# Query maxima from the transposed features, injected by full-mode matmuls, with keys and features in one block

## The reference, cut to what matters

```python
def _attn_ref(q, k, v, w_phi):              # batch 8, heads 8, seq 576, head_dim 64, 128 features
    def phi(x):
        proj = np.einsum('bhsd,df->bhsf', x, w_phi)
        proj = proj - np.max(np.abs(proj), axis=-1, keepdims=True)
        return np.concatenate([np.exp(proj), np.exp(-proj)], axis=-1)
    q_p, k_p = phi(q), phi(k)
    kv = np.einsum('bhsf,bhsd->bhfd', k_p, v)
    z = np.sum(k_p, axis=2)
    num = np.einsum('bhsf,bhfd->bhsd', q_p, kv)
    den = np.einsum('bhsf,bhf->bhs', q_p, z)[..., None] + 1e-06
    return num / den
# then, per batch, on the [576, 512] result x (fp32):
#   xk = mu_k*x + (1-mu_k)*x_prev;  xr = mu_r*x + (1-mu_r)*x_prev
#   x = sigmoid(xr @ w_r) * (relu(xk @ w_k)**2 @ w_v)
# and a second block: h = relu(x @ w_in); three-tap convolution along seq; h*sigmoid(conv) @ w_out
```

## Time and profile before

| | |
|---|---|
| median of 3 runs | 1417.46 us (1412.54 to 1421.47) |
| profiled execution, its own time | 1417.62 us |
| its span | 1415.8 us, 26326 instructions |
| TensorE busy | 1360.0 us, 96% |
| VectorE busy | 672.6 us, 48% |
| ScalarE busy | 626.6 us, 44% |
| DMA | 78.60 MB, mean 56 GB/s |

### The profile page before, as it was taken

One profiled execution on the slowest core, in us unless ns is written; L12 is line 12 of the kernel. 1 busy time (PEld: TensorE's weight loads), 2 busy tenths in 40 slices (PEclk: granted clock), 3 DMA queues, 4 the chain that ended last, 5 costly groups with the idle time before them and its releaser, 6 DMA issues. The chain is left out here.

```text
span 1415.8 us, 26326 instructions
## 1 busy us (share of the span) xinstructions
PE 1360.0 (96%) x10368; PEld 1211.6 (86%) x10368; DVE 672.6 (48%) x1047; ACT 626.6 (44%) x1111; POOL 13.5 (1%) x18
## 2 busy tenths in 40 slices
PE   5879999999999999999999999998899999999998
PEld 4668899889888889888988888998788988998997
DVE  5444244334433624442544362451757556655753
ACT  3536345454352534545445353443444443433532
POOL 0000000000000000000000000000300000000000
PEclk9879999999999999999999999999999999999999
DMA  5411202202212120220221212030310210110101
GB/s 165 124 45 40 58 27 77 63 20 69 61 45 70 40 58 26 62 78 19 70 54 53 69 41 58 25 116 22 93 64 1 71 64 30 41 63 30 41 30 38
DMA packets 94579, 78.60 MB, mean 56 GB/s; under 512 B 64656, under 2 KB 72976, under 8 KB 93456
## 3 DMA queue, kind: packets, MB, share of 16 engines
q1 hardware_dynamic: 94480, 77.10, 18.2%
HBM read 57.75 MB, written 19.02 MB: 54 GB/s over the span
## 5 line engine op out<-in xcount | busy, mean ns | idle before, releaser
L472 PE MATMUL psm<-xk_hi,wk_hi 128*128 128x288 f32 x512 | 158.6, 310 | 15.1 <-issue 6.9
L969 PE MATMUL psh<-y_hi,win_hi 128*128 128x288 f32 x512 | 153.9, 301 | 13.4 <-ACT h L1054 9.0
L818 DVE TENSOR_TENSOR k_lo<-square,k_hi 128x288 fp32r<-128x288 f32 x128 | 58.7, 458 | 221.3 <-ACT square L683 221.3
L472 PE MATMUL psm<-k_hi,wv_hi 128*128 128x288 f32 x512 | 154.4, 302 | 0.0
L472 PE MATMUL psm<-xk_lo,wk_hi 128*128 128x288 f32 x512 | 153.7, 300 | 0.0
L472 PE MATMUL psm<-xk_hi,wk_lo 128*128 128x288 f32 x512 | 153.2, 299 | 0.0
L970 PE MATMUL psh<-y_lo,win_hi 128*128 128x288 f32 x512 | 152.2, 297 | 0.0
L971 PE MATMUL psh<-y_hi,win_lo 128*128 128x288 f32 x512 | 151.6, 296 | 0.0
L472 PE MATMUL psm<-k_lo,wv_hi 128*128 128x288 f32 x512 | 151.1, 295 | 0.0
L472 PE MATMUL psm<-k_hi,wv_lo 128*128 128x288 f32 x512 | 150.8, 295 | 0.0
L1112 DVE SCALAR_TENSOR_TENSOR conv<-h,taps,conv 128x576 f32<-128x576 f32 x64 | 55.2, 863 | 141.3 <-ACT conv L1056 141.3
(11 more groups left out here) (116 smaller groups left out, 2810.9 us busy)
## 6 DMA issues: line engine op xcount, KB each, us to landing
v_nat<-in_v SPq DMA_DIRECT2D x32, 320.0 KB, 3.6
qk<-in_q SPq DMA_DIRECT2D x32, 288.0 KB, 2.9
qk<-in_k SPq DMA_DIRECT2D x32, 288.0 KB, 3.2
den<-den_scr SPq DMA_DIRECT2D x64, 144.0 KB, 3.0
y_scr<-y SPq DMA_DIRECT2D x64, 144.0 KB, 1.8
y<-y_scr SPq DMA_DIRECT2D x8, 1152.0 KB, 5.5
out<-rows SPq DMA_DIRECT2D x32, 256.0 KB, 2.0
den_parts<-den_rows SPq DMA_DIRECT2D x128, 2.2 KB, 1.9
```

The source lines that it names most:

```text
L472: return nc.tensor.matmul(o, lhsT, rhs, start=first, stop=last)
L818: nc.vector.tensor_tensor(k2_lo[:, i, :], square[:, i % 2, :], k2_hi[:, i, :].bitcast(F32), ALU.subtract).then_inc(k2_lo_ready, 1)
L969: nc.tensor.matmul(o, wh, xh, start=first, stop=False, skip_group_check=True)
```

## The change

The queries are projected once. The step E (`features_and_keys`) makes the query projections with features on partitions for all 576 tokens (four fp32 matmuls) and the key projections (ten), alternating between the two 64-row halves. VectorE turns the query features in 32x32 blocks (`q_turn`, two transposes) and reduces them to partial maxima (`part_maxima`); one TensorE transpose (M) brings the partial maxima of each token together, and VectorE reduces again and splits in hi and lo (`split_maxima`). Four DMAs on SP (`load_maxima`) lay the result out as rows, and the step PICK subtracts them by four f32r matmuls that use all 128 rows. The copy of the maxima by ScalarE and the second projection are gone. DEN and NUM write into the banks of the query features, in chunks of 512 and 64 columns; the key projections and KV use the other two banks. The steps' planned costs and fills are new, and the first batch no longer runs ahead into the second.

The diff, cut to its core:

```diff
-ROWS = D + 2
+TOK = S // 32
...
-PE_NS = {"QP": 1100, "KP": 1100, "M": 550, "P0": 800, "P1": 800, "KV": 2240, "DEN": 1000, "NUM": 1950,
+PE_NS = {"E": 2800, "M": 150, "PICK": 700, "KV": 4500, "DEN": 1200, "NUM": 2200,
          "K": 1590, "K-": 1190, "K+": 400, "R": 1590, "V-": 1590, "V": 1590}
 
-FILL_NS = {"QP": 2200, "M": 1600, "P0": 3500, "P1": 2600}
-FIRST_FILL, LAST_FILL, RC_AFTER, DV_AFTER = 6000, 1600, 3500, 9000
+FILL_NS = {"E": 3600, "M": 3200, "PICK": 1600, "KV": 1500, "NUM": 2200}
+FIRST_FILL, RC_AFTER, DV_AFTER = 6000, 3800, 9500
...
-    steps = [("QP", 0)]
-    for p in range(PAIRS):
-        steps += [(s, p) for s in ("KP", "M", "EK", "P0", "KV", "P1", "DEN", "NUM")]
-        steps += [("QP", p + 1)] if p + 1 < PAIRS else []
-    return steps
+    return [(s, p) for p in range(PAIRS) for s in ("E", "M", "EK", "PICK", "KV", "DEN", "NUM")]
...
-        def ahead(s):
-            return [(s, 0, "next") if last else (s, p + 1)]
-
         def before(s):
             return [(s, p - 1)] if p else []
 
-        steps += [("M", p)] + before("RC") + [("P0", p), ("EK", p)] + ahead("QP")
-        steps += [("KV", p), ("P1", p)] + before("DV") + ahead("KP") + [("DEN", p), ("NUM", p)]
+        steps += [("M", p)] + before("RC") + [("EK", p), ("PICK", p), ("KV", p)] + before("DV")
+        steps += [] if last else [("E", p + 1)]
+        steps += [("DEN", p), ("NUM", p)]
...
-            if not (ran_ahead and step in (("QP", 0), ("KP", 0))):
-                emit(step)
+            emit(step)
             if with_moe:
                 fill(FILL_NS.get(s, 0))
-                if s == "DEN":
+                if s == "NUM":
...
+    Q0, K_TAIL, Q_MAX, Q1 = 0, BANK + D, BANK + D + 2 * F, 2 * BANK - D
+    CHUNKS = (((0, BANK), (BANK, S)), ((0, D), (D, S)))
...
-    def await_att_psum(eng, p, a):
+    def q_cols(h, p, a):
+        return att_psum(p, a)[:, (Q0, Q1)[h]:(Q0, Q1)[h] + S]
+
+    def k_tail(p, a):
+        return att_psum(p, a)[:, K_TAIL:K_TAIL + 2 * F].rearrange("p (h f) -> p h f", h=2)
+
+    def k_main():
+        return ps1[:].rearrange("p h (t f) -> p h t f", t=TT - 1)
+
+    def turned_max(p, a):
+        return att_psum(p, a)[:, Q_MAX:Q_MAX + P]
+
+    def await_q_psum(eng, p, a):
 
         if first_of(a):
-            await_(eng, den_copied, PAIRS, a, p - 1)
+            await_(eng, num_copied, PAIRS, a, p - 1)
         elif second_of(a) and p == 0:
-            eng.wait_ge(den_copied, PAIRS - 1)
+            eng.wait_ge(num_copied, PAIRS - 1)
         else:
-            await_(eng, den_copied, PAIRS, a, p)
-
-    def place(h, t):
-        return (H - 1) * h + t
-
-    def blocks(flat):
-
-        return bass.AP(flat.tensor, flat.offset, [flat.ap[0], (F * (H - 1), 2), (F, TT), (1, F)])
-
-    def halves(flat):
-
-        return flat.rearrange("p (b s) -> p b s", s=BANK)[:, 0:2, 0:HALF]
+            await_(eng, num_copied, PAIRS, a, p)
...
+        def load_maxima(p, a):
+
+            await_(sp, q_max_split_ready, PAIRS, a, p + 1)
+            await_(sp, features, PAIRS, a, p)
+            for h in range(2):
+                for part in range(2):
+                    row = 2 * h + part
+                    sp.dma_start(max_rows[row:row + 1, :].bitcast(F32), q_max_split[TOK * h:TOK * h + TOK, part, :].bitcast(F32)).then_inc(rows_loaded, 16)
+
...
+                if kind == "M":
+                    load_maxima(step[1], a)
...
-                if kind == "DEN":
-                    spread_den(step[1], of)
+                if kind == "NUM":
+                    spread_den(step[1], a)
                 if kind == "RC":
-                    repeat_den(step[1], of)
+                    repeat_den(step[1], a)
...
-        def project(i, p, a):
-
-            if i == 0:
-                await_att_psum(pe, p, a)
-            else:
-                await_(pe, q_max_ready, PAIRS, a, p + 1)
-            await_(pe, (q_loaded, k_loaded)[i][p % 2], 16 * (PAIRS // 2), a, 16 * (p // 2 + 1))
-            ps = att_psum(p, a)
-            for n in range(TT):
-                for h, t in ((0, (n - 1) % TT), (1, (n + 1) % TT)):
-                    own, b = slice(D * h, D * h + D), place(h, t)
-                    if (h, t) == (1, 0):
-                        await_(pe, shared_bank, 2 * PAIRS, a, 2 * p + i + 1)
-                    last = mm(ps[:, F * b:F * b + F], qk[own, p % 2, i, P * t:P * t + P], phi[own, :], True, True)
-                    if (h, t) == (0, TT - 1):
-                        last.then_inc(shared_bank, 1)
-            last.then_inc(k_projected if i else q_projected, 1)
+        def features_and_keys(p, a):
+
+            await_q_psum(pe, p, a)
+            await_(pe, kvz_copied, PAIRS, a, p)
+            await_(pe, q_loaded[p % 2], 16 * (PAIRS // 2), a, 16 * (p // 2 + 1))
+            await_(pe, k_loaded[p % 2], 16 * (PAIRS // 2), a, 16 * (p // 2 + 1))
+            tails, keys = k_tail(p, a), k_main()
+
+            def key_tile(h, t):
+                own = slice(D * h, D * h + D)
+                o = tails[:, h, :] if t == TT - 1 else keys[:, h, t, :]
+                return mm(o, qk[own, p % 2, 1, P * t:P * t + P], phi[own, :], True, True)
+
+            def feature_chunk(h, chunk, first):
+                own, cols = slice(D * h, D * h + D), slice(*CHUNKS[h][chunk])
+                return mm(q_cols(h, p, a)[:, cols], phi[own, :], qk[own, p % 2, 0, cols], first, False)
+
+            key_tile(0, TT - 1).then_inc(shared_bank, 1)
+            feature_chunk(1, 1, True)
+            feature_chunk(0, 0, True)
+            await_(pe, shared_bank, 3 * PAIRS, a, 3 * p + 1)
+            key_tile(1, TT - 1).then_inc(shared_bank, 1)
+            key_tile(0, 0)
+            key_tile(1, 0)
+            await_(pe, shared_bank, 3 * PAIRS, a, 3 * p + 2)
+            feature_chunk(0, 1, True).then_inc(shared_bank, 1)
+            key_tile(1, 1)
+            key_tile(0, 1)
+            await_(pe, shared_bank, 3 * PAIRS, a, 3 * p + 3)
+            feature_chunk(1, 0, False).then_inc(raw_features, 1)
+            for t in range(2, TT - 1):
+                for h in range(2):
+                    last = key_tile(h, t)
+            last.then_inc(k_projected, 1)
 
         def turn_maxima(p, a):
-            await_(pe, q_max_split_ready, PAIRS, a, p + 1)
-            await_(pe, num_copied, PAIRS, a, p)
-            for t in range(TT):
-                last = nc.tensor.transpose(ps1[0:ROWS, P * t:P * t + P],
-                                           q_max_split[:, t, :, :].rearrange("p h r -> p (h r)")[:, 0:ROWS].bitcast(F32), ident[:])
-            last.then_inc(max_turned, 1)
-
-        def feature_rows(n, p, a):
-
-            if n == 0:
-                await_(pe, max_rows_ready, PAIRS, a, p + 1)
-            else:
-                await_(pe, q_exp_ready, 2 * H, a, 4 * p + 2)
-            cols = slice(HALF * n, HALF * n + HALF)
+            await_(pe, q_part_ready, PAIRS, a, p + 1)
+            nc.tensor.matmul(turned_max(p, a), q_part[:], ident[:], start=False, stop=True, is_transpose=True,
+                             skip_group_check=True).then_inc(max_turned, 1)
+
+        def subtract_maxima(p, a):
+            await_(pe, rows_loaded, 64 * PAIRS, a, 64 * (p + 1))
+            await_(pe, k_tail_shifted, PAIRS, a, p + 1)
...
+                for chunk in CHUNKS[h]:
+                    cols = slice(*chunk)
+                    last = mm(q_cols(h, p, a)[:, cols], pick[:, h, :], max_rows[:, cols], False, True)
...
-                        last = mm(ps1[D * h:D * h + D, BANK * n:BANK * n + HALF], kvz[:, h, e, 0:D], q_exp[:, e, h, cols],
-                                  e == 0, e == 1)
+                        last = mm(q_cols(0, p, a)[D * h:D * h + D, cols], kvz[:, h, e, 0:D], q_exp[:, e, h, cols], e == 0, e == 1)
...
-        def exp_q(n, p, a):
-            await_(act, features, H, a, 2 * p + n + 1)
+        def exp_q(p, a):
+            await_(act, features, PAIRS, a, p + 1)
             await_(act, attended, PAIRS, a, p)
-            for e in range(2):
-                nc.scalar.activation(q_exp[:, e, :, HALF * n:HALF * n + HALF], halves(ps1[:]), ACT.Exp,
-                                     scale=1.0 - 2.0 * e).then_inc(q_exp_ready, 1)
+            for h in range(2):
+                for e in range(2):
+                    nc.scalar.activation(q_exp[:, e, h, :], q_cols(h, p, a), ACT.Exp, scale=1.0 - 2.0 * e).then_inc(q_exp_ready, 1)
...
-            await_(act, den_summed, PAIRS, a, p + 1)
+            await_(act, attended, PAIRS, a, p + 1)
             await_(act, den_spread, 64 * PAIRS, a, 64 * p)
-            nc.scalar.activation(two(den_rows[:]), halves(att_psum(p, a)[:, BANK:3 * BANK]), ACT.Copy).then_inc(den_copied, 1)
+            nc.scalar.activation(den_rows[:], q_cols(1, p, a), ACT.Copy).then_inc(den_copied, 1)
 
         def copy_num(p, a):
             await_(act, attended, PAIRS, a, p + 1)
             await_(act, x_ready, PAIRS, a, p)
```

(64 more changed lines are left out.)

122 lines of the change are left out of this document (51 added, 71 removed).

## The result

The changed kernel takes **1660.1 us** (median of 4, 1656.93 to 1669.47); the one before, beside it, 1419.1 (median of 4, 1412.54 to 1421.47). The ratio is 1.172 (that of the two medians 1.170), with a 95% interval of 1.166 to 1.178. The profiled execution took 1656.93, its span 1655.0: 239.2 over the 1415.8 of before. The forecast was 1556, its range ended at 1612. The direction came as forecast, and so did the waits for the row loads; the size did not, above all because the clock was also low behind the shorter waits, which the forecast left out.

A forecast was written before the change was run, and what follows sets the result against it. The prediction took TensorE's work, busy 96% of the span, as the bound. 1417.6 + 89 (stalls less saving) + 41 (clock) + 8 (first batch) = 1556 us, chance 0.42; range 1472 to 1612.

The forecast's parts named there:

- TensorE's saving: Matrix work per pair falls from 13.1 to 11.6 us: 1.5 saved (bounds 1.0 to 2.1), 6.0 per woven iteration.
- 2.8 that had run ahead: Second batch's QP0 and KP0 formerly ran ahead in the first batch, saving iteration 0 2.8 us that was counted twice.
- The stalls: TensorE waits in each woven iteration, mostly before PICK: 18.7 us; against 6.0 saved, 12.7 longer, +89 over seven.
- kvz: In pair 0, DEN directly follows KV and waits for the copy of kvz and hand-overs: 0.6 us.
- K+00: At a woven iteration's end TensorE reaches this tile before its inputs are ready: stall 2.1 us with the hand-over.
- The term c: Time of the four row loads from SP's start: 3.7 us, bounds 2.3 and 4.5; stalls sum to 4c + 3.9.
- M's own split is long done: In pair 1, the maxima are split well before SP can start the row loads, which end at 12.7 us.
- VectorE's work: New VectorE operations per pair: transposes 0.75 us each, partial maxima 1.35, main keys 1.22, key tail 0.42.
- The clock: Half clock follows only the stalls of pairs 1 and 3, 2.9 us each: 5.8 per woven iteration, +41.
- the first rival: Clock also falls after the shorter stalls: two more 2.9 us stretches per woven iteration, +41, 1597; chance 0.13.
- The first batch: It ends 5.6 us later, at 100.0; with the time counted twice, +8.4 in all (bounds -4 and +20).
- 22 per pair: First-batch pair: E's end to PICK 4.8 plus 3.7 us, PICK through E 11, waits behind weight pieces 2.5.

The follow-up runs named there:

- combined kernel: Changed kernel with two row loads, a retuned step list, 14 matmuls in each first-batch wait and a reordered first batch: 1404.2 us, ratio 0.992 to the kernel before.
- List B: Changed kernel with two row loads and a step list with four tiles between M and PICK in most pairs, none between PICK and KV: 1514.35 us.

## Why the prediction was right in kind and short in size

Against 1556, 1656.93 is 101 too much. The terms, each in turn:

- **TensorE's saving**: nearly right. Per pair in the woven part of after, group start to group start at full clock: E 2.77 (forecast 2.5), M 0.03 (0.1), PICK 0.79 (0.67), KV 4.38 (4.50), DEN and NUM 3.18 (3.3); 11.15 against 11.1. By busy time the woven part saved 31.5, where the forecast had 39.2 (42 less the 2.8 that had run ahead). In the second iteration of the combined kernel TensorE is busy for 111.25 against 116.51 of before, 5.3 less and not 6.0. The rest was not followed.
- **The stalls**: right in place, order and nearly in size. Forecast before the four PICKs 3.0, 5.9, 2.8, 4.3; measured in the second iteration 3.41, 6.26, 4.05, 4.58. kvz 0.55 (0.6), K+00 2.5 (2.1). The term c was under-sized: from SP's first issue to PICK 4.14 to 4.20 instead of 3.7, as these issues take 0.76 to 0.78 each (293.45, 3.11 for four) where the spread's take 0.60. I carried over a duration of another shape: there one row goes out to 64 partitions, here 18 partitions come into one row. And "M's own split is long done" was tight: in pair 1 it ended 1.95 before the first issue and after TensorE had begun to wait. In all, idle rose by 147.1 where 7 x 18.7 = 131 was forecast.
- **VectorE's work**: right. The transposes take 762 ns each against the 754 of the row chosen, the partial maxima 1.33 (1.35), the keys 1.21 (1.22) and 0.39 (0.42).
- **The clock** is the step that failed: "I count these two and not the shorter: 5.8 per iteration, +41". Measured, 89.3. Two things were wrong in it. The stalls of 3 to 4 us, left out, also lowered the clock: behind 13 of the 14 in pairs 0 and 2 it was low for a while, for 81.6 us of busy time in all, which cost half of that, 41 (PICK of pair 2 in the second iteration, behind 4.05, took 1.45 instead of 0.79). That is what the first rival said, at 0.13, and its +41 came out for this part. And the 2.9 per stretch came from one row, and no case had another length: where the low stretch ran into KV it lasted up to 15.9 us. Behind pairs 1 and 3 it was low for 103.1 us, which cost 52 and not 41; the start of the woven part and the waits for xk_lo, 21.0 us, cost 10 more. The rival's 1597 is still 60 short, by this and by the terms below. List B shows the strongest case: a wait of 2.5 before KV, and KV at 8.4.
- **The first batch** failed as well: +5.6 forecast (the 2.8 that had run ahead is booked with the saving above), +28.35 measured. About 19 of it is clock: TensorE was busy at 0.50 for 58.1 us of this batch in after and for 20.0 in before. Two sizes did it, both in "22 per pair"; PICK came every 28.8, 29.7 and 26.2. "PICK, KV, kvz, E at partly half clock come to 11": from 18.79 to 33.75, pair 0's took 15.0, with KV at 9.1 where I had put the half clock on a part of it. And from E's end to the next PICK, forecast at 8.5 + 2.5, went 13.9 (33.75 to 47.60). The lists show why. VectorE in pair 1 of after:

```profile
39.22 1.23 DVE L744 TENSOR_TENSOR wk_lo<-diff,wk_hi 128x1024 fp32r<-128x1024 f32 x1 [1.71 <-ACT wk_hi L640]
40.36 0.28 DVE L762 TENSOR_REDUCE q_max<-psm 36x32 f32<-36x128 f32 x1
```

and SP there:

```profile
40.47 0.38 SPq L369 DMA_DIRECT2D diff<-in_moe_w_v  x1
40.89 2.46 SPq L386 DMA_DIRECT2D den_parts<-den_rows  x4
43.48 3.02 SPq L378 DMA_DIRECT2D max_rows<-q_max_split  x4
```

  M was done at 37, but VectorE's list has the split of a weight piece ahead of the second reduction, and SP's has the spread of the previous denominator (2.46) ahead of the loads. The second I had not counted in the first batch. In the combined kernel both are moved and the loads are two: from M to PICK went 4.35 in pair 2, and the 14 matmuls fill most of it; in after it was 10.62 there.
- **The last iteration and phase 2** have no term in the forecast: they took 5.95 more. 2.8 of it is a wait for xk_lo in the last iteration, which before did not have; 3.35 is longer busy time, at a granted clock of 0.98 instead of 0.99.

The miss as a sum: clock 48.3, waits 16.1, saving by busy time 7.7 (39.2 less 31.5), first batch 22.75 (28.35 less 5.6), end 5.95: 100.8.

The Trainium skill ("DMA: Bandwidth & Descriptors", Anatomy of one DMA) gives a DMA about 2.0 us of fixed cost, for GpSimd's path. With issues that cost next to nothing c would be an estimate of 2.2 by it. The rows of this case decide against that estimate for four DMAs of one queue: 3.11 go until the last issue is done, and PICK starts 1.1 after it.

## What to carry to other kernels

In this kernel a wait of the saturated TensorE cost its own length and, behind it, work at half clock; such a clock was seen behind waits from 1.8 us on. Price the second from what kind of work follows, and put dense tiles, not small fp32 matmuls, behind the wait: with one tile between, 6 of 28 KV ran wholly at half clock, with two none. When a step moves from an engine to DMAs, count the issues (here 0.7 to 0.8 us each, in order on the queue) and what stands ahead of them on that queue, and merge transfers: two loads instead of four took 78.8 us off. A list tuned to hide one chain has to be set anew with the change that replaces it: here the same change was 17% slower with its first order and 0.8% faster with another, two DMAs instead of four, and a few edits in the first batch.

## What the runs showed of the hardware that I had not expected

- The lower clock's stretch had no single length: 5.8 and 15.9 us behind waits of 6.26 and 4.67 with the same work after them. With two tiles of 288 columns ahead of KV's fp32 matmuls of 65 columns, the busy time at 0.50 in the woven part fell from 205.7 to 151.9 us, with the same waits before PICK. In the first batch of after, where KV follows PICK, all four KV took 9.1, in the combined kernel 5.05 to 5.10.
- Waits of 1.8 to 2.6 us were enough to lower the clock where KV stood right behind them: after all 14 in list B it was low, for 6.8 to 10.2 us.
- The issues on SP took different times for different shapes: 0.60 for one row to 64 partitions, 0.76 to 0.78 for 18 partitions to one row (3.11 for four), 0.70 for 36 partitions to two rows (1.40 for two).
- A 32x32 transpose on VectorE reads 576 fp32 columns from PSUM in 762 ns, as long as a multiplication of the same width (754).
